# Attention issued two steps at a time: scores, value products and flips in pairs, gate products ahead

## The chip, the cores and the metric

The kernel runs on one core of one Trainium2 chip. The metric is the device time of one execution in microseconds. Five engines work side by side and meet at semaphores: TensorE (matrix products, PE in the profile, its weight loads PEld), VectorE (DVE), ScalarE (ACT), GpSimd (POOL) and SyncE (SP), whose queue issues most of the loads.

## The reference

Three parts, each fed by the one before:

```python
# attention: q, k, v of (2, 8, 576, 64)
scores = scale * np.matmul(q, k.transpose(0, 1, 3, 2))
mask_local = (rel >= 0) & (rel < 32)                              # heads 0 to 3
mask_strided = (rel >= 0) & (pos[None, :] % 32 == pos[:, None] % 32)   # heads 4 to 7
attn = exp(scores - max); attn = attn / (sum + 1e-09)
x = matmul(attn, v), as (1152, 512)

# mixture 1: 8 experts, one for each token (argmax of gate logits)
logits = x @ w_gate + modality_bias[modality_id]
out[mask] = gate_w[mask, None] * (relu(x[mask] @ w1[e]) @ w2[e])

# mixture 2: 4 experts, all of them for each token, weighted
out += p[:, e:e + 1] * (relu(x @ w1[e]) @ w2[e])
```

## The kernel before

Attention is cut into 22 steps, 11 for each of two batches. A step covers four heads. Steps 0 to 4 of a batch are the strided heads: 126 queries by 126 keys of seven residues (72 by 72 in the fifth). Steps 5 to 10 are the local heads: 96 queries by 128 keys. One step goes through the engines like this:

- TensorE, `score(i)`: a mask product (L1412) fills one of three banks (1, 2, 3 in turn), then the products of queries and keys (L1417, two passes for each of four heads) add to it. It waits until the exponentials of step i-3 are done.
- VectorE: the maximum of each row (L993) and its negation (L995).
- ScalarE: four exponentials with their sums (L675) into one of four buffers `prob`.
- VectorE, `invert(m)`: sum plus 1e-9 (L944), reciprocal (L947).
- GpSimd: probabilities times the reciprocal (L509).
- TensorE, `flip_prob(m)`: four transposes (L1430) into bank 4 (even steps) or 5 (odd steps). ScalarE copies even ones out (`keep_prob`, L664), VectorE odd ones (L956). Each flip waits for the copy of the flip two steps before.
- TensorE, `weigh(m)`: value products (L1456), 64 columns of weights for each head, so that two heads write the lower and the upper half of the partitions of bank 6 or 7. VectorE copies the result to `xT` (`keep_att`, L979 and L984).

In the loop before (L1460 to L1468) each turn i issues the scores of step i, the flip of step i-3 (`LAG_T`) and the value products of step i-5 (`LAG_V`). The same order is written out by hand for the other engines: VectorE (L987 to L1015) takes the maximum of step i, then inverts the sum of step i-1, copies a flip if it is an odd one, copies the attention of step i-5. ScalarE (L666 to L681) copies an even flip, then takes the exponentials of step i.

Into this loop the kernel weaves the start of mixture 1. Once the tokens of tile t (128 tokens) are complete, the gate products of the tile (`gate_logits`, L1377, eight columns) are issued ahead of the value products of the same step, and a flip of the tile to token rows (`flip_rows`, L1372) behind them; `FLIP_AT` gives the step: tiles 0 to 3 at m = 8, 9, 10, 12. After step 10 VectorE finds the experts of the first three tiles, and at step 11 TensorE counts ranks (L1381 to L1393) and VectorE chooses the expert that is worked on first (`choose_first`). SyncE then asks for its weights (L388, L394), which ScalarE cuts (L650) right behind its last exponentials, ahead of the copy of flip 20. GpSimd scatters the rows of the three tiles (L503) behind the scalings of steps 17, 18 and 19; when all three have landed, SyncE loads the first tile of tokens of that expert (L408), and TensorE flips it (`flip_x`, L1499).

The remaining flips, value products and gate products (tiles 4 and 5) are written out behind the loop (L1470 to L1487). Ahead of the loop TensorE runs `WARM` = 8 products of ones (L1359). After attention come mixture 1 (L1522, L1536) and mixture 2 (L1612, L1641), which the change doesn't touch.

Of the kernel before, what the change touches and what calls it, by code (L numbers as in the profile page):

```python
# [40 lines left out]
def moe_chain(nc, qT_in, kT_in, v_in, modality_id, w_gate, modality_bias, w1, w2, domain_probs, u1, u2, out):  # L41
# [41 lines left out]
        return P if is_local(n) else residues(n) * PER_RES  # L83

    STEPS = B * TILES
    WARM, FIRST_TILES = 8, 2
    FIRST_COLS = FIRST_TILES * P_RES
    assert FIRST_TILES < STRIDED
    LAG_T, LAG_V = 3, 5
    PB = 4  # L90
    SCORE_BANKS = (1, 2, 3)

    def steps_before(t):

        b, at = divmod(P * (t + 1) - 1, S)
        return b * TILES + STRIDED + at // LQ + 1
# [1 line left out]

    GROUPS = ((0, 3), (3, 6), (6, 9))
    LOOP_TILES = GROUPS[1][0] + 1  # L100
    FLIP_AT, step = {}, 2 * STRIDED - 3
    for t in range(LOOP_TILES):
        step = max(step + (2 if t == 3 else 1), steps_before(t) + 1)
        FLIP_AT[step] = t
    FOUND_AT = max(step for step, t in FLIP_AT.items() if t < GROUPS[0][1])
    CHOSEN_AT = FOUND_AT + 1
    SCATTER_FROM = CHOSEN_AT + LAG_V + 1
    assert GROUPS[2][1] == NT and LOOP_TILES + 2 == GROUPS[1][1] and SCATTER_FROM + GROUPS[0][1] < STEPS

    ROW_BANK = [0] * LOOP_TILES + [2] * 3 + [1, 2]  # L110
# [49 lines left out]
    with ctx:  # L160
# [482 lines left out]
        def _(act):  # L643
# [19 lines left out]
                src = bank[4][:].rearrange("p (h r) -> p h r", h=HALF_H)  # L663
                a.copy(probT[0:C, 0, :, 0:R], src[0:C, :, 0:R]).then_inc(prob_kept_a, 1)  # L664

            for i in range(STEPS):  # L666
                m = i - LAG_T
                if m >= 0 and m % 2 == 0:
                    keep_prob(m)
                R, C, s = rows(i % TILES), keys(i % TILES), i % PB  # L670
                act.wait_ge(max_known, i + 1)
                if i >= PB:
                    act.wait_ge(prob_flipped, i - PB + 1)
                for h in range(HALF_H):
                    last = a.activation(prob[0:R, s, h, 0:C], bank[SCORE_BANKS[i % 3]][0:R, P * h:P * h + C], ACT.Exp,  # L675
                                        bias=neg_max[0:R, s, h:h + 1], scale=SCALE,
                                        accum_out=row_sum[0:R, s, h:h + 1])
                last.then_inc(exped, 1)
                t = FLIP_AT.get(i - LAG_V, 1)
                if t % 2 == 0:  # L680
                    keep_rows(t)  # L681

# [166 lines left out]
        def _(dve):  # L849
# [108 lines left out]
            def keep_att(m):  # L958

                b, n = divmod(m, TILES)  # L960
                R = rows(n)
                dve.wait_ge(weighed, m + 1)
                if m in FLIP_AT:
                    t = FLIP_AT[m]
# [22 lines left out]
            for i in range(STEPS):  # L987
                if i == TILES + 2:
                    small_steps()
# [7 lines left out]
                if i >= 1:  # L997
                    invert(i - 1)
                m = i - LAG_T
                if m >= 0 and m % 2:  # L1000
                    keep_prob(m)
                m = i - LAG_V
                if m >= 0:
                    keep_att(m)
                if m == FOUND_AT:
                    dve.wait_ge(vstep, st.value)
                    find_experts(slice(*GROUPS[0]))
                if m == CHOSEN_AT:
                    choose_first()
                if m == CHOSEN_AT + 1:  # L1010
                    find_slots(slice(*GROUPS[0]))
                if m == CHOSEN_AT + 2:
                    place_first()
                if FLIP_AT.get(m, 0) % 2:
                    keep_rows(FLIP_AT[m])  # L1015

            keep_prob(STEPS - 3)
            keep_att(STEPS - 5)
            invert(STEPS - 1)
            keep_att(STEPS - 4)  # L1020
# [3 lines left out]
            find_experts(slice(*GROUPS[1]))  # L1024
            keep_prob(STEPS - 1)
            for m in range(STEPS - 3, STEPS):
                keep_att(m)


            def keep_xt(j):  # L1030
# [324 lines left out]
        def _(pe):  # L1355
# [78 lines left out]
            def weigh(m):  # L1434

                b, n = divmod(m, TILES)
                R, C = rows(n), keys(n)
                pe.wait_ge(prob_kept_v if m % 2 else prob_kept_a, m // 2 + 1)
                if n == 0 or n == STRIDED:
                    pe.wait_ge(v_read[b][is_local(n)], 16)  # L1440
                if m >= 2:
                    pe.wait_ge(att_kept, m - 1)
                if m in FLIP_AT:
                    pe.wait_ge(gate_in, 16)
                    gate_logits(FLIP_AT[m], bank[6 + m % 2][:, P * 2:P * 2 + E])
# [8 lines left out]
                for h in range(HALF_H):  # L1454
                    o = D * (h % 2)
                    last = t_.matmul(bank[6 + m % 2][o:o + D, P * (h // 2):P * (h // 2) + R],  # L1456
                                     v_rows[0:C, m, h, :], probT[0:C, m % 2, h, 0:R], start=True, stop=True)
                last.then_inc(weighed, 1)

            for i in range(STEPS):  # L1460
                score(i)
                if i >= LAG_T:
                    flip_prob(i - LAG_T)
                m = i - LAG_V
                if m >= 0:
                    weigh(m)
                if m in FLIP_AT:
                    flip_rows(FLIP_AT[m], bank[0])  # L1468

            flip_prob(STEPS - 3)  # L1470
            weigh(STEPS - 5)
# [3 lines left out]
            flip_rows(LOOP_TILES, bank[ROW_BANK[LOOP_TILES]])  # L1475
            flip_prob(STEPS - 2)
            weigh(STEPS - 4)
            pe.wait_ge(att_kept, steps_before(LOOP_TILES + 1))
            gate_logits(LOOP_TILES + 1, bank[3][:, E:2 * E]).then_inc(logit_done, 1)
            flip_prob(STEPS - 1)  # L1480
            weigh(STEPS - 3)
            flip_rows(LOOP_TILES + 1, bank[ROW_BANK[LOOP_TILES + 1]])
            weigh(STEPS - 2)
            t0, t1 = GROUPS[1]
            pe.wait_ge(onehot_ready, 2)
            rank_group(t0, t1, bank[3][:, 2 * E:(2 + t1 - t0) * E]).then_inc(rank_done, 1)
            weigh(STEPS - 1)  # L1487


            def rank_last():  # L1490
# [259 lines left out]
```

## Time and profile before

| | |
|---|---|
| median of 3 runs | 608.01 us (607.55 to 608.05) |
| profiled execution | 611.28 us, span of the core 609.5 us |
| TensorE busy | 600.8 us, 99% of the span |
| VectorE, ScalarE, GpSimd busy | 347.3, 219.0, 300.8 us |
| attention on TensorE | from 5.27 to about 62 us |

A row of the timeline gives start, duration, engine, line, operation, what it writes and reads, the count, and in brackets the idle time before it and what ended that. A row of the chain of work that ended last gives start, duration and what. A row of a stretch gives its bounds and length, then for each engine the busy time and the number of instructions, the granted clock of TensorE (1.00 is 2.4 GHz, 0.50 is 1.2 GHz), the busy share of the DMA engines and GB/s.

### The profile page before, as it was taken

What the parts mean: (1) busy time and instruction counts of PE and PEld (TensorE: products, weight loads), DVE (VectorE), ACT (ScalarE), POOL (GpSimd) and SP (SyncE); (2) the same over time, 40 slices, a digit from 0 to 9 for tenths busy, and PEclk for the clock granted to TensorE, in tenths of its full rate; (3) what the DMA queues carried; (4) which work ended last, traced back from release to release, by engine and by line L of the source; (5) the groups of instructions that cost most, each with busy time, mean ns of one, the idle gap of its engine ahead of it and who ended that gap; (6) DMA issues with size and microseconds to landing.
All of it is one profiled execution on the core that took longest, in us unless ns stands there. A gap on an engine that the chain in (4) does not pass through costs nothing.

```text
span 609.5 us, 10253 instructions
## 1 busy us (share of the span) xinstructions
PE 600.8 (99%) x3615; PEld 527.5 (87%) x3616; DVE 347.3 (57%) x714; ACT 219.0 (36%) x543; POOL 300.8 (49%) x286
## 2 busy tenths in 40 slices
PE   8999999999999999999999999999999999999996
PEld 6898878888878889989889899899899899899894
DVE  6888775248882123785454554554554554654553
ACT  7867532258973231223123123122132132131130
POOL 5537301541100009449996945846756747646005
PEclk9999799999999999999999999999999999999999
DMA  8817446629951002002222112112112011020004
GB/s 233 226 47 277 159 174 238 210 84 306 351 221 30 24 17 70 1 0 70 70 69 71 35 35 69 36 35 69 33 36 69 24 45 60 12 65 0 0 0 155
DMA packets 25116, 56.83 MB, mean 93 GB/s; under 512 B 6784, under 2 KB 7808, under 8 KB 25088
## 3 DMA queue, kind: packets, MB, share of 16 engines
q1 hardware_dynamic: 16656, 32.06, 15.9%
q0 software_dynamic: 6848, 21.52, 10.9%
q10 hardware_dynamic: 1584, 2.88, 1.6%
q8 instruction: 16, 0.26, 0.2%
q14 instruction: 12, 0.10, 0.1%
HBM read 49.10 MB, written 7.36 MB: 93 GB/s over the span
## 4 chain that ended last, share of the span: by engine, by line
PE 86%; DMA 3%; DVE 3%; POOL 3%; issue 2%; ACT 1%; DVEq 0%; SPq 0%; ACTq 0%; POOLq 0%
PE bank L1641 30%; PE bank L1612 30%; PE bank L1522 8%; PE bank L1536 8%; PE bank L1417 2%; DMA w_raw<-in_moe_w 2%; POOL out L637 1%; PE bank L1456 1%; PE bank L1377 1%; PE bank L1511 1%; PE bank L1430 1%; PE bank L1372 1%; DVE w_lo L937 1%; PE bank L1499 1%; PE bank L1412 1%
## 5 line engine op out<-in xcount | busy, mean ns | idle before, releaser
L1277 DVE SCALAR_TENSOR_TENSOR acc<-bank,meta_s,acc 128x512 f32<-128x512 f32 x135 | 100.8, 748 | 62.2 <-PE bank L1641 62.1
L1641 PE MATMUL bank<-u_hi,h_hi 128*128 128x512 f32 x288 | 112.3, 390 | 0.0
L1641 PE MATMUL bank<-u_lo,h_hi 128*128 128x512 f32 x288 | 112.1, 389 | 0.0
L1641 PE MATMUL bank<-u_hi,h_lo 128*128 128x512 f32 x288 | 112.0, 389 | 0.0
L1324 DVE SCALAR_TENSOR_TENSOR h_lo<-bank,h_hi 128x288 fp32r<-128x288 f32 x112 | 50.9, 455 | 44.7 <-ACT h_hi L825 22.9
L1612 PE MATMUL bank<-x2T_hi,u_hi 128*128 128x288 f32 x232 | 68.4, 295 | 0.0
L1612 PE MATMUL bank<-x2T_lo,u_hi 128*128 128x288 f32 x232 | 68.4, 295 | 0.0
L1612 PE MATMUL bank<-x2T_hi,u_lo 128*128 128x288 f32 x232 | 68.3, 295 | 0.0
L813 ACT COPY part_p<-bank 128x288 f32<-128x288 f32 x28 | 11.2, 400 | 157.9 <-PE bank L1612 157.9
L1612 PE MATMUL bank<-t_hi,u_hi 128*128 128x288 f32 x224 | 66.2, 295 | 0.0
L1612 PE MATMUL bank<-t_lo,u_hi 128*128 128x288 f32 x224 | 66.0, 295 | 0.0
L1612 PE MATMUL bank<-t_hi,u_lo 128*128 128x288 f32 x224 | 65.9, 294 | 0.0
L1641 PEld LDWEIGHTS bank<-u_hi,h_lo 128*128 128x128 f32 x288 | 54.1, 188 | 11.4
L1641 PEld LDWEIGHTS bank<-u_hi,h_hi 128*128 128x128 f32 x288 | 54.1, 188 | 10.1
L1641 PEld LDWEIGHTS bank<-u_lo,h_hi 128*128 128x128 f32 x288 | 54.1, 188 | 10.0
L584 POOL TENSOR_TENSOR u_lo<-u_raw,u_hi 128x1792 fp32r<-128x1792 f32 (+1 forms) x16 | 61.6, 3852 | 1.3
L574 POOL TENSOR_TENSOR u_raw<-u_raw 128x256 f32<-128x256 f32 x14 | 10.3, 735 | 87.7 <-PE bank L1612 71.0
L554 POOL DMA_INDIRECT meta_by_rank<-meta,pos x9 | 11.5, 1273 | 84.2 <-ACT y_tile L710 61.9
L582 POOL CAST u_hi<-u_raw 128x1792 fp32r<-128x1792 f32 (+1 forms) x16 | 25.6, 1601 | 41.3 <-PE bank L1612 38.2
L1612 PEld LDWEIGHTS bank<-x2T_hi,u_hi 128*128 128x128 f32 x232 | 43.5, 188 | 0.7 <-issue 0.2
L1612 PEld LDWEIGHTS bank<-x2T_lo,u_hi 128*128 128x128 f32 x232 | 43.5, 188 | 0.6
L1612 PEld LDWEIGHTS bank<-x2T_hi,u_lo 128*128 128x128 f32 x232 | 43.5, 188 | 0.0
(237 smaller groups left out, 1234.0 us busy)
## 6 DMA issues: line engine op xcount, KB each, us to landing
w_raw<-in_moe_w SPq DMA_DIRECT2D x20, 1024.0 KB, 8.5
u_raw<-in_moe_w POOLq DMA_DIRECT2D x16, 512.0 KB, 3.8
u_raw<-in_moe_w POOLq DMA_DIRECT2D x16, 256.0 KB, 3.2
u_raw<-in_moe_w POOLq DMA_DIRECT2D x32, 128.0 KB, 2.9
x_tile<-x_by_expert ACTq DMA_DIRECT2D x11, 256.0 KB
x_by_expert<-zero_row SPq DMA_DIRECT2D x10, 256.0 KB, 2.7
qT<-in_qT SPq DMA_DIRECT2D x3, 576.0 KB, 6.3
kT<-in_kT SPq DMA_DIRECT2D x6, 288.0 KB, 7.3
```

The source lines that it names most:

```text
L554: pool.indirect_dma_start(out=ms, out_offset=bass.IndirectOffsetOnAxis(ap=pos[:, t:t + 1], axis=0), in_=meta[:, t, :], in_offset=None).the ...
L574: g.tensor_tensor(u1_raw[:, S1], u1_raw[:, A21], u1_raw[:, A22], ALU.add).then_inc(u_summed, 1)
L582: g.tensor_copy(u1_hi[n % 2][:, need], u1_raw[:, need]).then_inc(u1_hi_cut, 1)
L584: g.tensor_tensor(u1_lo[n % 2][:, need], u1_raw[:, need], u1_hi[n % 2][:, need].bitcast(FP32), ALU.subtract)\
L813: a.copy(part[s][k][:], bank[s][:, 0:SUB]).then_inc(part_kept[s], 1)
L1277: w.scalar_tensor_tensor(out=acc[:, t, :], in0=bank[Z_BANK[i]][:], scalar=meta_s[:, t, bass.ds(e + 1, 1)], in1=acc[:, t, :], op0=ALU.mult, ...
L1324: w.scalar_tensor_tensor(out=h_lo[:, i, cols_of(s, k)], in0=bank[at][:, 0:SUB], scalar=0.0, in1=h_hi[:, i, cols_of(s, k)].bitcast(FP32), o ...
L1417: last = t_.matmul(bank_s[0:R, h, 0:C], qT[:, b, c, q0:q0 + R], kT[:, b, h % 2, c, k0:k0 + C], start=False, stop=True, skip_group_check=True)
L1522: last = t_.matmul(bank[half][:], lhs[:, c, :], rhs[:, c, HALF * half:HALF * (half + 1)], start=c == 0 and lhs is xt_hi and rhs is w1_hi, ...
L1536: last = t_.matmul(bank[5][:], lhs[:, f, :], rhs[:, f, :], start=f == 0 and rhs is w2_hi and lhs is ht_hi, stop=f == FCH - 1 and lhs is ht_lo)
L1612: last = t_.matmul(bank[at][:, 0:SUB], lhs_part[page][:, lhs, c, :], rhs[:, c, :], start=start and c == 0 and i == 0, stop=c == KC - 1 and ...
L1641: last = t_.matmul(bank[Z_BANK[i]][:], lhs[:, c, ts], rhs[page][:, c, :], start=c == 0 and k == 0, stop=c == 1 and k == 2)
```

## The change

Everything in the attention loop goes by two steps. TensorE issues the scores of steps i and i+1, then the gate products of steps m and m+1 (m = i-4), then the value products of both, then the flip of a tile to rows if one is due, then the flips of steps i-2 and i-1. `LAG_T` becomes 2, `LAG_V` 4. In the turn with m = 0 the two flips stand between the scores of steps 4 and 5. VectorE takes the maxima of steps i and i+1 first, then copies and inverts; ScalarE takes the exponentials of both, then copies an even flip. Gate products have steps of their own (`GATE_AT`: tiles 0 to 3 at 8, 9, 10, 12), flips to rows others (`ROWS_AT`: 8, 10, 12, 14). The ranks of the first group move from step 11 to step 12, the scatters stay behind the scalings of steps 17 to 19. `WARM` becomes 10.

```diff
-    WARM, FIRST_TILES = 8, 2
+    WARM, FIRST_TILES = 10, 2
-    LAG_T, LAG_V = 3, 5
+    LAG_T, LAG_V = 2, 4
...
+    CHOSEN_AT = FOUND_AT - FOUND_AT % 2 + 2
...
 (ScalarE)
+            for i in range(0, STEPS, 2):
+                exponential(i)
+                exponential(i + 1)
+                if i >= LAG_T:
+                    keep_prob(i - LAG_T)
+                t = ROWS_AT.get(i - LAG_V, 1)
                 if t % 2 == 0:
                     keep_rows(t)
...
 (VectorE)
+            for i in range(0, STEPS, 2):
+                find_max(i)
+                find_max(i + 1)
                 m = i - LAG_V
+                if m == min(GATE_AT) - min(GATE_AT) % 2:
+                    small_steps()
                 if m >= 0:
                     keep_att(m)
+                if m == CHOSEN_AT:
+                    choose_first()
+                invert(i)
+                if m >= 0:
+                    keep_att(m + 1)
+                if i >= LAG_T:
+                    keep_prob(i - LAG_T + 1)
+                invert(i + 1)
+                if m == FOUND_AT - FOUND_AT % 2:
                     dve.wait_ge(vstep, st.value)
                     find_experts(slice(*GROUPS[0]))
                 if m == CHOSEN_AT:
                     find_slots(slice(*GROUPS[0]))
                     place_first()
...
 (TensorE)
+            for i in range(0, STEPS, 2):
+                m = i - LAG_V
                 score(i)
+                if m == 0:
                     flip_prob(i - LAG_T)
+                    flip_prob(i - LAG_T + 1)
+                score(i + 1)
                 if m >= 0:
+                    if m >= 2:
+                        pe.wait_ge(att_kept, m)
+                    gates(m)
+                    gates(m + 1)
                     weigh(m)
+                    weigh(m + 1)
+                if m in ROWS_AT:
+                    flip_rows(ROWS_AT[m], bank[0])
+                if i >= LAG_T and m != 0:
+                    flip_prob(i - LAG_T)
+                    flip_prob(i - LAG_T + 1)
+
             pe.wait_ge(exped, STEPS - 1)
             pe.wait_ge(att_kept, steps_before(LOOP_TILES))
             gate_logits(LOOP_TILES, bank[3][:, 0:E])
             pe.wait_ge(att_kept, steps_before(LOOP_TILES + 1))
             gate_logits(LOOP_TILES + 1, bank[3][:, E:2 * E]).then_inc(logit_done, 1)
+            flip_prob(STEPS - 2)
+            flip_rows(LOOP_TILES, bank[ROW_BANK[LOOP_TILES]])
+            weigh(STEPS - 4)
+            weigh(STEPS - 3)
             flip_prob(STEPS - 1)
             flip_rows(LOOP_TILES + 1, bank[ROW_BANK[LOOP_TILES + 1]])
             weigh(STEPS - 2)
+            weigh(STEPS - 1)
```

## Rows read from the trace of the kernel before

**Rows 1.** Busy time by stretch, behind attention.
```profile
100.00:150.00 50.00, 50.00 (x250) 40.95 (x249) 24.38 (x28) 27.13 (x41) 18.63 (x18) 1.00 0.67 225
```

**Rows 2.** Chain of work that ended last, one local step.
```profile
26.46 0.48 PE bank L1456 x8
26.94 0.36 PE bank L1412
27.30 0.88 PE bank L1417 x8
28.18 0.33 PE bank L1430 x4
```

**Rows 3.** The same chain, other widths, gate products and a flip of rows.
```profile
22.37 0.58 PE bank L1456 x8
...
24.50 0.40 PE bank L1456 x8
...
32.60 0.82 PE bank L1377 x8
...
33.91 0.59 PE bank L1372 x4
34.49 0.21 PE bank L1412
```

**Rows 4.** The same chain at the start of attention.
```profile
9.78 0.69 DVE row_max L993
...
10.70 1.51 ACT prob L675 x8
...
12.69 1.04 POOL prob L509
...
18.76 0.35 PE bank L1412
```

**Rows 5.** Timeline at the start, ScalarE and VectorE.
```profile
8.57 0.37 ACT L675 ACTIVATE prob<-bank,neg_max 126x126 f32<-126x126 f32 x1 [2.47 <-DVE neg_max L995]
...
12.12 0.37 ACT L675 ACTIVATE prob<-bank,neg_max 126x126 f32<-126x126 f32 x1
...
12.53 0.65 DVE L993 TENSOR_REDUCE row_max<-bank 126x4 f32<-126x504 f32 x1
...
13.50 0.59 ACT L664 COPY probT<-bank 126x504 f32<-126x504 f32 x1
```

**Rows 6.** Timeline of TensorE at the start.
```profile
1.03 3.59 PE L1359 MATMUL bank<-ones 128*128 128x512 bf16 x8 [1.03 <-POOL ones L449]
5.27 0.65 PE L1412 MATMUL bank<-mask_res,ident_b 126*126 126x504 bf16 x1 [0.64 <-DMA kT<-in_kT]
5.71 1.91 PE L1417 MATMUL bank<-kT,qT 128*126 128x126 f32 x8
...
9.95 1.08 PE L1417 MATMUL bank<-kT,qT 128*126 128x126 f32 x8
```

**Rows 7.** Granted clock by stretch, last but two columns, end of attention.
```profile
64.00:65.00 1.00, 1.00 (x8) 0.97 (x8) 1.00 (x2) 0.34 (x1) 0.84 (x1) 0.82 1.02 389
...
71.00:72.00 1.00, 1.00 (x11) 0.63 (x11) 0.00 (x0) 1.00 (x2) 0.00 (x0) 0.77 0.00 0
```

**Rows 8.** Timeline at the end of attention, all engines.
```profile
55.21 0.55 PE L1430 MATMUL bank<-ident,prob 96*128 96x96 f32 x4 [0.46 <-POOL prob L509]
...
55.32 1.01 POOL L503 DMA_INDIRECT x_by_expert<-xtok,slot  x1 [0.17 <-issue]
...
61.12 0.36 SPq L408 DMA_DIRECT2D x_tile<-x_by_expert  x1
...
63.55 0.96 PE L1377 MATMUL bank<-gate,xT 128*128 128x8 f32 x8
...
64.16 1.09 POOL L503 DMA_INDIRECT x_by_expert<-xtok,slot  x1 [2.94 <-DMA x_tile<-x_by_expert]
...
65.23 1.06 PE L1499 MATMUL bank<-ident,x_tile 128*128 128x128 f32 x4
```

More of the change, by code:

```diff
@@ L100, in moe_chain @@
     LOOP_TILES = GROUPS[1][0] + 1
-    FLIP_AT, step = {}, 2 * STRIDED - 3
+    GATE_AT, ROWS_AT, step = {}, {}, STRIDED
     for t in range(LOOP_TILES):
[L103 to L106, printed above, removed]
+        step = step + 1
+        while step - step % 2 < steps_before(t):
+            step = step + 1
+        GATE_AT[step] = t
+    for t in range(LOOP_TILES):
+        first = min(step for step, u in GATE_AT.items() if u == t)
+        ROWS_AT[max(first - first % 2, max(ROWS_AT, default=0) + 2)] = t
+    FOUND_AT = max(step for step, t in GATE_AT.items() if t < GROUPS[0][1])
+    CHOSEN_AT = FOUND_AT - FOUND_AT % 2 + 2
     SCATTER_FROM = CHOSEN_AT + LAG_V + 1
+    assert STEPS % 2 == 0 and STRIDED == LAG_V + 1
     assert GROUPS[2][1] == NT and LOOP_TILES + 2 == GROUPS[1][1] and SCATTER_FROM + GROUPS[0][1] < STEPS
@@ L664, in keep_prob, with exponential @@
                 a.copy(probT[0:C, 0, :, 0:R], src[0:C, :, 0:R]).then_inc(prob_kept_a, 1)
[L666 to L669, printed above, removed]
+            def exponential(i):
                 R, C, s = rows(i % TILES), keys(i % TILES), i % PB
@@ L678, in _ @@
                 last.then_inc(exped, 1)
-                t = FLIP_AT.get(i - LAG_V, 1)
+            for i in range(0, STEPS, 2):
[4 more added lines that the diff above has]
+                t = ROWS_AT.get(i - LAG_V, 1)
                 if t % 2 == 0:
@@ L962, in keep_att @@
                 dve.wait_ge(weighed, m + 1)
-                if m in FLIP_AT:
-                    t = FLIP_AT[m]
+                if m in GATE_AT:
+                    t = GATE_AT[m]
                     w.tensor_tensor(logits[:, t, :], bank[6 + m % 2][:, P * 2:P * 2 + E], bias_tok[:, 0, t, :],
@@ L985, in keep_att, with find_max @@
                     last.then_inc(att_kept, 1)
-            for i in range(STEPS):
-                if i == TILES + 2:
-                    small_steps()
+            def find_max(i):
                 R, C, s = rows(i % TILES), keys(i % TILES), i % PB
@@ L996, in _ @@
                  .then_inc(max_known, 1)
[L997 to L1001, printed above, removed]
+            for i in range(0, STEPS, 2):
+                find_max(i)
+                find_max(i + 1)
                 m = i - LAG_V
+                if m == min(GATE_AT) - min(GATE_AT) % 2:
+                    small_steps()
                 if m >= 0:
                     keep_att(m)
-                if m == FOUND_AT:
+                if m == CHOSEN_AT:
[7 more added lines that the diff above has]
+                if m == FOUND_AT - FOUND_AT % 2:
                     dve.wait_ge(vstep, st.value)
@@ L1008, in _ @@
                 if m == CHOSEN_AT:
-                    choose_first()
-                if m == CHOSEN_AT + 1:
                     find_slots(slice(*GROUPS[0]))
-                if m == CHOSEN_AT + 2:
                     place_first()
[L1014 to L1020, printed above, removed]
+                if ROWS_AT.get(m, 0) % 2:
+                    keep_rows(ROWS_AT[m])
             dve.wait_ge(logit_done, 1)
@@ L1024, in _ @@
             find_experts(slice(*GROUPS[1]))
+            keep_att(STEPS - 4)
+            keep_att(STEPS - 3)
             keep_prob(STEPS - 1)
-            for m in range(STEPS - 3, STEPS):
-                keep_att(m)
+            keep_att(STEPS - 2)
+            keep_att(STEPS - 1)
             def keep_xt(j):
@@ L1442, in weigh, with gates @@
                     pe.wait_ge(att_kept, m - 1)
-                if m in FLIP_AT:
+                for h in range(HALF_H):
+                    o = D * (h % 2)
+                    last = t_.matmul(bank[6 + m % 2][o:o + D, P * (h // 2):P * (h // 2) + R],
+                                     v_rows[0:C, m, h, :], probT[0:C, m % 2, h, 0:R], start=True, stop=True)
+                last.then_inc(weighed, 1)
+            def gates(m):
+                if m in GATE_AT:
                     pe.wait_ge(gate_in, 16)
-                    gate_logits(FLIP_AT[m], bank[6 + m % 2][:, P * 2:P * 2 + E])
+                    gate_logits(GATE_AT[m], bank[6 + m % 2][:, P * 2:P * 2 + E])
                 if m == CHOSEN_AT:
@@ L1453, in weigh @@
                     count_group(t1, bank[6 + m % 2][:, at:at + E])
[L1454 to L1460, printed above, removed]
+            for i in range(0, STEPS, 2):
+                m = i - LAG_V
                 score(i)
-                if i >= LAG_T:
+                if m == 0:
                     flip_prob(i - LAG_T)
-                m = i - LAG_V
+                    flip_prob(i - LAG_T + 1)
+                score(i + 1)
                 if m >= 0:
+                    if m >= 2:
+                        pe.wait_ge(att_kept, m)
+                    gates(m)
+                    gates(m + 1)
                     weigh(m)
[L1467 to L1471, printed above, removed]
+                    weigh(m + 1)
[4 more added lines that the diff above has]
+                    flip_prob(i - LAG_T + 1)
             pe.wait_ge(exped, STEPS - 1)
@@ L1474, in _ @@
             gate_logits(LOOP_TILES, bank[3][:, 0:E])
-            flip_rows(LOOP_TILES, bank[ROW_BANK[LOOP_TILES]])
-            flip_prob(STEPS - 2)
-            weigh(STEPS - 4)
             pe.wait_ge(att_kept, steps_before(LOOP_TILES + 1))
             gate_logits(LOOP_TILES + 1, bank[3][:, E:2 * E]).then_inc(logit_done, 1)
+            flip_prob(STEPS - 2)
+            flip_rows(LOOP_TILES, bank[ROW_BANK[LOOP_TILES]])
+            weigh(STEPS - 4)
+            weigh(STEPS - 3)
             flip_prob(STEPS - 1)
-            weigh(STEPS - 3)
             flip_rows(LOOP_TILES + 1, bank[ROW_BANK[LOOP_TILES + 1]])
             weigh(STEPS - 2)
+            weigh(STEPS - 1)
             t0, t1 = GROUPS[1]
@@ L1486, in _ @@
             rank_group(t0, t1, bank[3][:, 2 * E:(2 + t1 - t0) * E]).then_inc(rank_done, 1)
-            weigh(STEPS - 1)
             def rank_last():
```

## The prediction

> **What bounds the kernel now.** I read the busy time by stretch first, then the chain of work that ended last, then the timelines of the stretches that the change touches, then the granted clock. In the stretch from 100 to 150 us TensorE is busy for all of it [rows 1], the first of ten such stretches up to 600 us, which read alike, so a microsecond won before is won at the end. Attention covers 5.3 to some 62 us. There TensorE is busy without a break from 14 to 54 us. It waits at the start, where the first softmax has to run through VectorE, ScalarE and GpSimd, and once at 55.2 us, for 0.46 us, for GpSimd [rows 8]. So two things decide: what TensorE needs for a pair of steps, and whether the other engines keep up with the new order.
>
> **What a step costs.** In the chain a step without gate work is mask product, score products, flip, value products: 0.36 + 0.88 + 0.33 + 0.48 = 2.05 us [rows 2]. Value products take 0.40 us for 72 columns, 0.48 for 96 and 0.58 for 126 [rows 2, 3]. That is a line of 3.3 ns a column with 0.16 us left at zero columns: a fixed cost on entering them. The mask product takes 0.36 us behind value products [rows 2] but 0.21 behind a flip of rows (the row at 34.49, [rows 3]): 0.14 to 0.15 for leaving them. Value products write halves of the partitions (64 columns of weights each), all else uses the full width. By the Trainium skill, page "TensorEngine Tiling (Array Packing)", section "Tiling Modes", a change of tiling mode drains the engine. The trace agrees as far as it goes: 0.16 us in and 0.14 out. If that rule alone were at work, two value products of one mode in a row would share one drain.
>
> **The change part by part.**
> 1. Pairs of value products. Before, 22 steps each enter and leave: 22 x 0.30. After, 11 pairs do: 11 x 0.30 = **3.3 us saved** on TensorE. No row shows two value products of different steps in a row, so the bounds are 0 (the cost is one of a step, not of a mode) and 3.3. I take 3.3, since eight products of one step with alternating halves show no such cost among themselves.
> 2. Start, at the clock of before. VectorE now takes the maxima of two steps and then inverts two sums. The second inversion waits for the exponentials of step 1, and the maximum of step 2 is queued behind it. Exponentials of step 1 start at 10.70 and are done at 12.21; the inversion ends at about 12.53, which is when the maximum of step 3 started before [rows 4, 5]. So now the maximum of step 2 starts at 12.53. With 0.69 + 0.18 + gaps, exponentials of step 2 start at 13.45 (before 12.12), those of step 3 1.42 later at 14.87 (the spacing 10.70 to 12.12), and are done at 16.4. Only then does ScalarE copy the first flip out (0.59, [rows 5]), which flip 2 needs: flip 2 runs 16.9 to 17.35. GpSimd scales step 3 from 16.75 to 17.8 (1.04, [rows 4]), flip 3 (0.43) ends at 18.3, scores of step 5 at 19.35, value products 0 and 1 (0.16 + 0.42 + 0.42) at 20.35. Before, the value products of step 1 ended at 18.76 with the scores of step 6 (0.35 + 0.88) done too, thus 17.53 for the same work [rows 4]. Start costs 2.8, and one saved mode change is in it: **3.1 us of waits added**. Bounds 2.3 to 3.6, by whether the copy of the first flip really ends the wait.
> 3. Middle. VectorE and ScalarE form a loop now: maximum and negation 0.88, exponentials of two steps 1.42 + 1.51, inversion 0.3, and only then the next maximum: 4.1 us a pair. TensorE needs 2 x (0.21 + 0.88 + 0.32 + 0.33) + 0.30 = 3.8 for a pair without gate work. So the pairs gain less than they seem to, as long as they run on the slack between score and flip; pairs with gate products and flips of rows (0.82 + 0.59 more, [rows 3]) refill it. No wait taken here.
> 4. End. In the iteration of step 16 VectorE does ranks, slots and places of the first group, and the maximum of step 18 is queued behind. Count from the end of scores 17, as estimates from the durations above: value products 12 end at 1.7, VectorE has copied and chosen by 3.3, inverted 16 and 17 and copied by 4.9, and is free at 6.1. Exponentials 18 run 7.0 to 8.4, 19 to 9.9; TensorE has ended scores 21 at 9.8 and wants flip 19 at about 11.7, when the scaling of 19 is held by that of 18 and a scatter (1.0 + 1.2 on GpSimd) until 12.1. So 0.4 of waiting; then 0.3 for exponentials 20 before the gate product that uses the scores' bank, and 0.2 for a copied row tile: 0.9, against the 0.46 of before [rows 8], which goes. **0.45 added**, bounds -0.5 to 1.2.
> 5. The first token tile. Its load is issued at 61.12, after the third scatter (issued 55.32) has landed, GpSimd sees it at 64.16, and TensorE reaches its flip at 65.23 [rows 8]: 1.1 us of slack. The scatters keep their place behind the scaling of steps 17 to 19. These come some 1.0 to 1.5 us later by parts 2 and 4, so the tile becomes the last to arrive: **0.3 added**, bounds 0 to 1. The expert's weights are asked for later as well, by the same delay. On ScalarE the first cut of them stands ahead of the copy of flip 20, so a late weight would hold value products 20. The trace of before shows ScalarE never waiting there, so I put it at nothing; it is in the upper bound.
> 6. Gate products ahead of the value products, flips behind: the same instructions in another place, inside the count of part 1; the mode changes are the same. Zero.
> 7. Ten products of ones. Eight run from 1.03 for 3.59 us at 0.43 us each, half clock, and TensorE then sits for 0.64 us until keys arrive at 5.27 [rows 6]. Two more fill just that hole and end at 5.3 to 5.5: nothing is delayed by more than 0.2. The level granted here is read from the durations: products of step 0 take 1.91 us for eight, those of step 2 only 1.08 from 9.95 on [rows 6]. So the engine went from 1.2 to 2.4 GHz near 9.9, after work without a break from 5.27. Without the hole it works without a break from 1.03, and the rise may come sooner: at best before the first score (5.3), at worst at 9.9 as now. I take 6.5, in the scores of step 0. They end 0.64 sooner, exponentials of step 0 start at 7.93 instead of 8.57 [rows 5], those of step 1 1.42 later, at 9.35 instead of 10.70: **1.3 saved**, bounds 0 and 1.9 (all scores at 2.4 GHz).
> 8. The clock in the new lull. By part 2 TensorE has, between the scores of step 4 and flip 3, some 3 us with one flip of 0.43 in it. In the trace the clock falls to 0.50 in the stretch 64 to 65 and is back in 71 to 72: some 6.8 us at 1.2 GHz, worth 3.4 [rows 7]. What TensorE did before that fall shows as busy, but the most of it is gate products with eight columns each, 0.96 us for a tile [rows 8]. The lull is thinner than that. Its price lies between 0 (no fall, or a slow stretch that ends with the lull) and 3.4 (one like that at the end, all under dense work). I take a fall that costs about half of it, since a part lies in the waits: **1.6 added**.
>
> Sum: -3.3 + 3.1 + 0.45 + 0.3 - 1.3 + 1.6 = **+0.85 us**. The profiled execution took 611.28 us with a span of 609.5, the median of the runs is 608.01. The profiled one should go to about 612.1, the median to **608.85**.
>
> **The rivals.**
> A. The clock rises early and stays: the same sum without part 8, 608.85 - 1.6 = 607.25. For it: there are some short flips in the lull. Against: the lull holds fewer columns than the stretch before 64.7.
> B. Slower: no early rise (eight products of ones, 3.59 us without a break, didn't bring it, and two more may not, [rows 6]) and a fall in the lull: 608.85 + 1.3 = 610.15. It decides as soon as products of step 1 still take 1.7 us and those of step 5 twice 0.88. Without rise and without fall it is 608.55.
> C. The fall at the end goes. The slow stretch at the end costs 3.4 [rows 7]. With attention packed more closely around 61 to 64 us it may be kept: 605.45. Against: products for the gate of tiles 6 and 7 stand where they stood, and in the new tail two more stand side by side.
> D. The change doesn't do what it says: entering and leaving cost something per step, and half of the 3.3 stays: 608.85 + 1.65 = 610.5.
>
> **How the numbers follow.** Forecast 0.33, A 0.26, B with fall 0.12, neither rise nor fall 0.08, C 0.14, D 0.07. Stalls of parts 2, 4 and 5 are known to about 0.8 us around each. 0.2% is 1.2 us, about what a measurement of this kernel can tell from no change. Slower than 609.2: a third of the forecast, B, D and a little of the others, 0.33. Faster than 606.8: C and a third of A, 0.24. The rest, 0.43, within. The range goes from 606.2 (A with its spread) to 610.6 (B and D), which leaves out C and little else.
>
> **What would show it.** Mode changes: the mask product of odd steps at 0.21 and one entry cost for each pair. Start: TensorE waits between the scores of step 4 and flip 3, over 2 us in all, released by ScalarE's copy and by GpSimd, and VectorE's maximum of step 2 starts behind the inversion of step 1. Clock: products of step 1 near 0.9 us for eight (early rise), scores of steps 5 to 7 near twice their time (fall). End: the flip of the first token tile released by its load. If the waits at the start come to less than 1.5 us, or the clock is high from 6.5 to 64 us, I am wrong on the slow side.

## The result and the profile after

The changed kernel takes **615.57 us** in the median of four executions (614.62 to 616.23), the kernel before 607.78 beside it: a ratio of 1.0123, 95% interval 1.0103 to 1.0143. It is slower by 7.8 us, where 608.85 and a range up to 610.6 were forecast. The profiled execution took 614.62 us with a span of 612.9. TensorE is busy for 597.9 us, 98% of the span, against 600.8 and 99% of a shorter one; VectorE, ScalarE and GpSimd are busy for about as long as before (350.6, 217.8, 301.6 us).

TensorE's waits up to 75 us, of the kernel after. The columns are the engine, what it wrote, the line, what ended the wait, then the sum in us, how often, and the longest; `issue` means that the profile shows nothing that the engine waited for.

```profile
PE bank L1443 <- ACT probT L670: 2.2, 1, 2.2
PE bank L1443 <- POOL prob L515: 1.8, 4, 0.7
PE bank L1425 <- ACT prob L679: 1.3, 1, 1.3
PE bank L1458 <- issue: 1.1, 3, 0.5
...
PE bank L1390 <- ACT prob L679: 1.0, 1, 1.0
PE bank L1425 <- DMA kT<-in_kT: 0.4, 1, 0.4
```

These six come to 7.8 us. The same view of the kernel before has only two, beside the 1.0 us for the ones that both kernels have:

```profile
PE bank L1430 <- POOL prob L509: 0.8, 2, 0.5
PE bank L1412 <- DMA kT<-in_kT: 0.6, 1, 0.6
```

So 6.4 us of waits came in, and the saving in mode changes (3.3) pays half of them. The start, on TensorE's timeline after (it answers to [rows 6]):

```profile
1.03 4.45 PE L1372 MATMUL bank<-ones 128*128 128x512 bf16 x10 [1.03 <-POOL ones L455]
...
5.70 1.18 PE L1430 MATMUL bank<-kT,qT 128*126 128x126 f32 x8
...
12.29 0.65 PE L1443 MATMUL bank<-ident,prob 126*126 126x126 f32 x4 [0.67 <-POOL prob L515]
...
15.80 0.69 PE L1443 MATMUL bank<-ident,prob 126*126 126x126 f32 x4 [2.21 <-ACT probT L670]
16.76 1.10 PE L1443 MATMUL bank<-ident,prob 126*126 126x126 f32 x4 [0.27 <-POOL prob L515]
...
18.08 1.80 PE L1430 MATMUL bank<-kT,qT 128*96 128x128 f32 x8
```

The products of the first score take 1.18 us where they took 1.91: the clock rose early. Flip 2 waits 2.21 us for ScalarE's copy, as forecast. The products of 18.08 take 1.80, twice the 0.88 of [rows 2]: the clock has fallen. The end, on the same timeline (it answers to [rows 8]):

```profile
56.77 0.42 PE L1425 MATMUL bank<-mask_local,ident_b 96*96 96x512 bf16 x1 [1.27 <-ACT prob L679]
...
58.57 0.88 PE L1458 MATMUL bank<-probT,v_rows 128*64 128x96 f32 x16 [0.51 <-issue]
...
60.55 0.55 PE L1443 MATMUL bank<-ident,prob 96*128 96x96 f32 x4 [0.62 <-POOL prob L515]
62.11 1.95 PE L1390 MATMUL bank<-gate,xT 128*128 128x8 f32 x16 [1.01 <-ACT prob L679]
...
72.01 0.60 PE L1523 MATMUL bank<-ident,x_tile 128*128 128x128 f32 x4
```

Four waits of 3.41 us stand where there was one of 0.46, and the flip of the first token tile starts at 72.01 instead of 65.23. Granted clock by stretch, after (columns as in [rows 7]):

```profile
17.00:18.00 1.00, 1.00 (x5) 0.93 (x5) 0.00 (x0) 1.00 (x8) 0.00 (x0) 0.50 1.19 226
...
64.00:65.00 1.00, 1.00 (x7) 1.00 (x7) 0.83 (x3) 0.75 (x1) 1.00 (x2) 0.50 0.92 369
65.00:66.00 1.00, 1.00 (x10) 0.67 (x10) 0.58 (x4) 0.00 (x0) 0.91 (x4) 0.50 0.11 41
```

There are two slow stretches, from about 16.2 to 19.6 us and from 64.0 to 67.4. Besides, every profile of this study, before and after, is at 0.50 in the last 1 to 4 us of its span.

**A quantity for what follows.** How long the clock stays low differs between executions of one kernel, so I set two numbers beside each time: the granted clock, averaged over the span, and the span times that clock. The product takes out what the low clock adds and leaves work and waits. It is a rough tool: the clock is given to three digits, which is 0.3 us either way; where TensorE waits at the low clock it takes out too much; and the slow products of ones at the start are still in it, since the clock reads 1.00 there. Medians:

| kernel | executions | time, us | clock | span x clock, us |
|---|---|---|---|---|
| before (beside the first experiments) | 31 | 608.65 | 0.997 | 605.2 |
| after | 4 | 615.57 | 0.992 | 608.9 |

The kernel after wasn't repeated; the four executions of before beside it had a median of 607.78. Of the 7 us or so between the two rows, 3.7 are work and waits (6.4 of waits less 3.3 of mode changes is 3.1), and the rest, some 3.2, is the lower clock: 613.8 x 0.008 = 4.9 us against 606.9 x 0.003 = 1.8.

### The profile page after: what moved, and what is told of

Its sections match the earlier page's. It is cut to its first block, busy times and chain, and to the rows that moved or that the text cites. A ratio compares the mean times of both kernels' runs of the same rounds, so it can differ in the third digit from the quotient of the medians.

```text
span 612.9 us, 10261 instructions
## 1 busy us (share of the span) xinstructions
PE 597.9 (98%) x3617; PEld 525.7 (86%) x3618; DVE 350.6 (57%) x714; ACT 217.8 (36%) x543; POOL 301.6 (49%) x286
## 4 chain that ended last, share of the span: by engine, by line
PE 88%; DVE 4%; ACT 2%; POOL 2%; issue 1%; DMA 1%; SPq 0%; POOLq 0%
PE bank L1665 30%; PE bank L1636 29%; PE bank L1560 10%; PE bank L1546 10%; ACT prob L679 2%; PE bank L1535 2%; POOL out L643 1%; PE bank L1430 1%; PE bank L1458 1%; PE bank L1523 1%; DVE row_max L1002 1%; PE bank L1529 1%; PE bank L1443 1%; PE bank L1372 1%; PE bank L1390 1%
```

## The experiments

**The kernel before, once more.** Unchanged.

> The kernel before once more, unchanged, for a second profile and the span and clock of several executions. The median of the runs of before is 3.3 us under its profiled execution (608.0 against 611.3). Theory 'slow tail': the profiled one had a stretch at 1.2 GHz behind attention (64 to 72 us, worth 3.4 us) that most executions don't have; then this profile, or most of its runs, shows a span near 606 and a clock above 0.995. Rival 'profiling costs it': the span is 609.5 again with the same slow stretch.

Measured: 608.88 us, ratio 1.0005 (0.998 to 1.003), and a profile with a span of 606.1 us, 3.4 less than the profiled execution that the prediction was worked from. The two stretches of [rows 7] and the flip of the token tile read:

```profile
64.00:65.00 1.00, 1.00 (x10) 0.97 (x10) 1.00 (x2) 0.31 (x1) 0.73 (x1) 1.00 0.97 365
71.00:72.00 1.00, 1.00 (x6) 0.81 (x5) 0.99 (x2) 0.86 (x2) 0.73 (x1) 1.00 0.00 0
...
64.92 0.60 PE L1499 MATMUL bank<-ident,x_tile 128*128 128x128 f32 x4
```

The slow tail that I took for a fixed cost of the kernel (3.4 us, part 8 and rival C) is absent here. Two thirds of the executions of before have a clock of 0.996 or more. So the 3.3 us between the profiled 611.28 and the median 608.01 were mostly this stretch.

**Ten products of ones alone** (kernel before with `WARM = 10`).

```
-    WARM, FIRST_TILES = 8, 2
+    WARM, FIRST_TILES = 10, 2
```

> The kernel before with ten products of ones instead of eight, nothing else. Theory of the forecast: the clock rises in the scores of step 0, the first exponentials start 0.7 to 1.3 us sooner, and the whole kernel gains 1.3: ratio 0.998. Rival: the loads of queries and keys hold the third score, and the start is given back: ratio 1.000.

Measured: 607.55 us, ratio 0.9974 (0.9952 to 0.9996); span x clock 604.2. A gain of 1.0 us by span x clock and 1.6 by the ratio, against 1.3 forecast: part 7 is right as far as this can tell, the interval being 0.2 to 2.9 us. In the profiled execution the products of each of the first four scores take 1.04 us, and the third waits 0.95 us for its keys (the first 0.66: the hole of part 7 isn't filled, as the ten products of ones take only 4.07 us there), so only part of the early rise comes through. It is the fastest kernel of the study, by little more than can be told.

**The second inversion behind the next pair's first maximum** (kernel after).

```
                 find_max(i)
+                if i >= 2:
+                    invert(i - 1)
                 find_max(i + 1)
...
-                invert(i + 1)
...
+            invert(STEPS - 1)
```

> The changed kernel; VectorE takes the second inversion of a pair behind the first maximum of the next pair, so the maximum no longer waits for the exponentials. Theory 'loop' (VectorE and ScalarE go round in 4.1 to 4.5 us a pair): the waits in the middle and half of those at the start and the end go, 3 to 4 us of 7.8; about 612. Rival 'clock' (the loss is slow stretches): 615.5, with the same slow stretches in the profile.

Measured: 609.83 us, ratio 1.0021 (0.9999 to 1.0044); span x clock 605.1, clock 0.9955. This one move takes 5.7 us off the median (6.2 by the ratios), where 3 to 4 and a time of 612 were expected. Of them 3.8 are work and waits, as expected for the loop; the other 2 are clock (0.9955 against 0.992). VectorE in the middle of attention, after:

```profile
22.74 0.66 DVE L1002 TENSOR_REDUCE row_max<-bank 96x4 f32<-96x512 f32 x1
23.43 0.53 DVE L1004 TENSOR_SCALAR neg_max<-row_max 96x4 f32<-96x4 f32 x1
...
26.91 0.17 DVE L954 TENSOR_SCALAR row_sum<-row_sum 96x4 f32<-96x4 f32 x1
27.20 0.65 DVE L1002 TENSOR_REDUCE row_max<-bank 96x4 f32<-96x512 f32 x1
```

The maximum of 27.20 starts 4.46 us after that of 22.74, right behind the second inversion (from 26.91), which waits for exponentials that wait for the maximum before: a closed loop, which I had put at 4.1. ScalarE is idle in it 1.2 to 1.3 us a pair. The missing 0.36 is one small operation, at 23.43, that takes 0.53 instead of 0.17. It ends at 23.96, and GpSimd's scaling that was under way ends at 22.90 + 1.04 = 23.94: it didn't run slowly but was held until the scaling was done. GpSimd's scalings show this and the period, first after and then with the deferred inversion:

```profile
22.90 1.04 POOL L515 TENSOR_TENSOR prob<-prob,row_inv 96x512 f32<-96x512 f32 x1 [0.61 <-DVE row_inv L957]
...
25.98 1.04 POOL L515 TENSOR_TENSOR prob<-prob,row_inv 96x512 f32<-96x512 f32 x1 [2.04 <-DVE row_inv L957]
...
30.44 1.04 POOL L515 TENSOR_TENSOR prob<-prob,row_inv 96x512 f32<-96x512 f32 x1 [2.04 <-DVE row_inv L957]
```

```profile
25.85 1.04 POOL L515 TENSOR_TENSOR prob<-prob,row_inv 96x512 f32<-96x512 f32 x1 [1.10 <-DVE row_inv L957]
...
29.87 1.04 POOL L515 TENSOR_TENSOR prob<-prob,row_inv 96x512 f32<-96x512 f32 x1 [1.28 <-DVE row_inv L957]
```

The period of 4.46 became 4.02, and the wait of 2.21 at the start became 0.83.

**Ten more products of ones in the lull** (kernel after; ahead of flip 2).

```
                 if m == 0:
+                    for _ in range(10):
+                        t_.matmul(bank[7][:].rearrange("p (h c) -> p h c", h=HALF_H), ones[:],
+                                  ones[:].unsqueeze(1).to_broadcast([P, HALF_H, P]), start=True, stop=True)
                     flip_prob(i - LAG_T)
```

> The changed kernel with ten more products of ones (0.21 us each) between the scores of step 4 and the flip of step 2, where TensorE waits 2.2 us. Theory 'clock falls in the lull': the level stays at 1.00 from 16 to 20 us and 1.6 us come back, about 614. Rival: the clock falls whatever the lull holds, or another fall takes its place: 615.5.

Measured: 614.94 us, ratio 1.0084 (1.0049 to 1.012); span x clock 608.7 as without them, clock 0.9935 against 0.992. In the profile the granted clock is 1.00 in every stretch from 14 to 22 us, so the fall in the lull is gone. The second slow stretch stays. The times tell its price badly: 0.6 us by the medians, 0.9 by the clock (613.8 x 0.0015), 2.4 by the ratios (1.0084 against 1.0123), with six executions that spread over 2.9 us. The two profiles tell more. GpSimd's scalings of steps 3 and 4, after and then with the filled lull:

```profile
15.68 1.03 POOL L515 TENSOR_TENSOR prob<-prob,row_inv 126x504 f32<-126x504 f32 x1 [0.36 <-DVE row_inv L957]
21.62 0.67 POOL L515 TENSOR_TENSOR prob<-prob,row_inv 72x288 f32<-72x288 f32 x1 [4.92 <-DVE row_inv L957]
```

```profile
16.11 1.03 POOL L515 TENSOR_TENSOR prob<-prob,row_inv 126x504 f32<-126x504 f32 x1 [0.36 <-DVE row_inv L957]
20.65 0.67 POOL L515 TENSOR_TENSOR prob<-prob,row_inv 72x288 f32<-72x288 f32 x1 [3.52 <-DVE row_inv L957]
```

Step 3 is 0.43 us later with the filled lull (keys came later), step 4 is 0.97 earlier: the fall costs 1.4 us here, and 0.95 of the lead is still there at the last scaling (62.98 against 63.93). This execution then loses 1.0 us to loads of weights in mixture 1, which stand on its chain of work at 153 and 166 us and not on that of the kernel after. Part 8 was right that the lull brings a fall, and its price of 1.6 fits the profiles; the medians can't settle it.

**Slots and places behind the next pair's maxima** (kernel after).

```
                 find_max(i + 1)
                 m = i - LAG_V
+                if m == CHOSEN_AT + 2:
+                    find_slots(slice(*GROUPS[0]))
+                    place_first()
...
-                if m == CHOSEN_AT:
-                    find_slots(slice(*GROUPS[0]))
-                    place_first()
```

> The changed kernel with slots and places of the first group taken one iteration later on VectorE, behind the maxima of steps 18 and 19. Theory 'queue': in the changed kernel these stand 2.3 us ahead of the maximum of step 18, and the waits of TensorE before scores 21 (1.27) and value products 16 (0.51) come from them; they go, 1.2 to 1.8 us, span times clock 607.3 instead of 608.9. Rival 'loop only' (VectorE and ScalarE set the pace anyway): under 0.5 us.

Measured: 616.63 us, ratio 1.011 (1.0045 to 1.0176); span x clock 607.55, 1.35 below after and near the expected 607.3, but clock 0.9875. In the profile the wait of 1.27 is gone and a flip waits 1.20 instead of 0.62, so the waits at the end sum to 2.72 instead of 3.41; the wait of 0.51, which was expected to go, stays. Where the rest of the 1.35 comes from isn't shown. A longer slow stretch (61 to 71 us) took more than that back. By the time alone one would have called the move useless.

**Both deferrals**, twice, on two occasions.

> Both edits on VectorE: second inversion behind the next maximum, and slots and places one iteration later. If the two causes add, span times clock is 1 us under that of the deferred inversion alone (605.1): 604.1, and the ratio to before about 0.999. Rival: with the loop gone the slots hide already, no difference to the deferred inversion alone.

Measured: 610.42 us, ratio 1.0018 (0.9984 to 1.0051), span x clock 604.9. Second occasion:

> The changed kernel with both deferrals, once more, on the chip of the two kernels with the extra products of ones: 610.4 as before, granted clock 0.994 in the median. If the clock of its executions is 0.997 or more here, the fall depends on the chip and the hour and the two kernels beside it say nothing on its cause.

Measured: 611.12 us, 1.0039 (1.002 to 1.0058), 605.1. Beside the deferred inversion alone (605.1) the slots give nothing, as the rival had it. Work and waits are back at those of before (604.4 to 605.2), and what is left of 2.5 to 3 us is the clock, 0.993 to 0.994 against 0.997. But back at before isn't below it: the 3.3 us saved on mode changes and the 1.0 of the early rise are still eaten by waits. In the first profile TensorE waits for other engines or keys for 4.5 us up to 75 us (0.70, 0.82, 0.69 and 1.06 at flips among them), against 1.4 before. So even with both deferrals the change gains nothing.

**A tiny full-width product between two value products** (both deferrals, nine pairs).

```
                     weigh(m)
+                    t_.matmul(bank[6 + (m + 1) % 2][:, 480:488], ones[:], ones[:, 0:8], start=True, stop=True)
                     weigh(m + 1)
```

> The kernel with both VectorE edits, and in each of the nine pairs of value products inside the loop one product of ones with 8 columns at full width between the two steps. Theory 'mode': each breaks a pair and brings back 0.30 us plus 0.03 for itself, 9 x 0.33 = 3.0 us where TensorE has no wait to hide it, 2 us or more in all. Rival 'cost per step': the two value products paid their 0.16 separately already, and only some 0.3 us are added in all.

Measured: 610.89 us, ratio 1.0046 (1.0019 to 1.0073); span x clock 605.6, so 0.7 above the same kernel without it, where 2 or more were expected. The chain of work shows the price itself, first without and then with the product, both at 96 columns:

```profile
29.71 0.81 PE bank L1460 x16
```

```profile
29.47 0.48 PE bank L1460 x8
29.95 0.11 PE bank L1491
30.07 0.48 PE bank L1460 x8
```

Sixteen value products take 0.81, or 0.48 + 0.11 + 0.48 = 1.07 with a product of eight columns between: some 0.27 more a pair with the small product's own time in it, 2.4 for nine, and 0.48 is what a step cost before [rows 2]. Only 0.7 of that reaches the end. The rest went into waits for GpSimd, as far as the profiles show: TensorE's weight loads wait 4.8 us for scalings up to 57 us in both profiles without the products and 2.9 with them, and the two flips behind the pair shown take 0.81 us with and 1.02 without.

**The second tile's gate products behind two value products** (both deferrals).

```
             gate_logits(LOOP_TILES, bank[3][:, 0:E])
-            pe.wait_ge(att_kept, steps_before(LOOP_TILES + 1))
-            gate_logits(LOOP_TILES + 1, bank[3][:, E:2 * E]).then_inc(logit_done, 1)
...
             weigh(STEPS - 3)
+            pe.wait_ge(att_kept, steps_before(LOOP_TILES + 1))
+            gate_logits(LOOP_TILES + 1, bank[3][:, E:2 * E]).then_inc(logit_done, 1)
```

On VectorE the copies of value products 18 and 19 go ahead of the logits to fit.

> Both VectorE edits, and in the written-out end the gate products of tile 5 stand behind value products 18 and 19 instead of right behind those of tile 4, with the two copies ahead of the logits on VectorE. Theory 'thin stretch': the clock falls at 60 us because two gate products stand side by side with waits around them; spread out it falls less often, more of the runs have a clock of 0.996 or more than with both edits alone, median 1 us lower. Rival: the falls come from the flips of rows and gate products of tiles 6 to 8, where nothing is changed: same share of low clocks.

Measured: 617.33 us, ratio 1.0107 (1.0064 to 1.015), and a span x clock of 604.8, the same as without the move. The clock is 0.982. Its profile is at half clock from about 57.6 to 78 us, of which this is one stretch:

```profile
70.00:71.00 1.00, 1.00 (x6) 1.00 (x7) 0.00 (x0) 0.33 (x1) 0.93 (x1) 0.50 0.67 258
```

The time is some 7 us longer with span x clock unchanged: the clock alone moves this kernel as far as the whole change did. That the clock falls less when these thin products are spread out is refuted for this order.

**Products of ones in the waits at the end** (both deferrals, on the second occasion). Four of 512 columns between flips 18 and 19; the second kernel has six more of 384 columns between the gate products of the two tiles.

```
                     flip_prob(i - LAG_T)
+                    if i == STEPS - 2:
+                        for _ in range(4):
+                            t_.matmul(bank[5][:].rearrange("p (h c) -> p h c", h=HALF_H), ones[:],
+                                      ones[:].unsqueeze(1).to_broadcast([P, HALF_H, P]), start=True, stop=True)
                     flip_prob(i - LAG_T + 1)
...
             gate_logits(LOOP_TILES, bank[3][:, 0:E])
+            for _ in range(6):
+                t_.matmul(bank[3][:, P:].rearrange("p (h c) -> p h c", h=3), ones[:],
+                          ones[:].unsqueeze(1).to_broadcast([P, 3, P]), start=True, stop=True)
```

> The changed kernel with both deferrals (inverses and slots behind the next pair's first maximum), and four extra products of ones of 512 columns (0.22 us each, 0.88 in all) in the wait of 1.06 us that TensorE has between the flips of steps 18 and 19. Question: is the slow stretch from about 58.5 to 62 us brought on by TensorE's waits just ahead of it? If the waits bring it on: the granted clock stays at 1.00 from 57 to 63 us, the median of the granted clock rises from 0.994 to 0.998, and the time falls by 1.5 to 2 us against the same kernel without them, to some 608.5. If the gate products with eight columns bring it on, and not the waits: same clock, time the same or up to 0.3 later.

Measured: 609.75 us, 1.0028 (1.001 to 1.0046), clock 0.996 in the median against 0.993 without. Against the kernel without the products the clock rose by 0.003 and the time fell by 1.4 us, where 0.004 and 1.5 to 2 were expected if the waits bring the fall on, and nothing if they don't.

> As the one with four products, and six more products of ones of 384 columns (0.16 us each, about 1.0 us) between the gate products of the first and of the second tile behind attention. If waits or thin gate products bring the clock down, it stays at 1.00 from 57 to 66 us; the six products stand on the path, so the time is 608.5 + 1.0 = 609.5 where the four alone suffice, and still some 609.5 (against 610.4 without either) where only both together keep the clock. If the fall has nothing to do with what TensorE does there: the slow stretch is as long as before, and the time is 610.4 + 1.0 = 611.4.

Measured: 609.92 us (609.18 to 610.4), 1.0008 (0.9983 to 1.0033), clock 0.997. All ten executions are at 0.996 or more; of the same kernel without the products, on the same chip, not one of ten is. Span x clock rose from 605.1 to 606.4, the 1.0 us of the six products, and still the median fell from 611.12 to 609.92. The two sets of clocks don't overlap (0.997 to 0.999 against 0.992 to 0.995); the times do (609.18 to 610.4 against 609.33 to 612.08). TensorE by stretch, in the kernel with neither, with four, with ten; the columns are the bounds, length, busy time and count of TensorE, granted clock, DMA share, GB/s:

```profile
55.00:57.00 2.00, 0.93 (x13) 1.00 0.98 323
57.00:59.00 2.00, 2.00 (x18) 0.80 1.01 365
59.00:61.00 2.00, 2.00 (x12) 0.50 1.01 386
...
63.00:65.00 2.00, 2.00 (x16) 0.50 0.16 24
```

```profile
55.00:57.00 2.00, 1.80 (x17) 1.00 0.95 322
57.00:59.00 2.00, 2.00 (x21) 1.00 1.00 356
...
67.00:69.00 2.00, 2.00 (x13) 0.81 1.05 408
69.00:71.00 2.00, 2.00 (x8) 0.50 0.60 233
```

```profile
57.00:59.00 2.00, 2.00 (x18) 1.00 1.03 360
...
69.00:71.00 2.00, 2.00 (x28) 1.00 0.56 210
```

Without them TensorE waits half of the two microseconds from 55 to 57 and the clock falls at once behind. With the wait filled it doesn't fall there. With four alone it falls later, near 68; with ten not at all in this execution.

## Why the prediction was wrong

The forecast was +0.85 us and the time moved by some 7. Three steps failed. Part 3 took no wait for the loop of VectorE and ScalarE. Part 4, which should have inherited the loop's lag, put 0.45 us where the waits at the end grew by 2.95. And part 8 with the sum carried the slow stretch at the end as something that doesn't change, though the median of before hasn't got it and the kernel after has.

**Part 1, mode changes: right.** The value products of two steps of 126 columns enter once (1.01 = 0.16 + 0.84), and the mask product of an odd step takes 0.22 instead of 0.36. From the chain of work after:

```profile
20.89 0.35 PE bank L1425
21.24 0.87 PE bank L1430 x8
22.11 0.22 PE bank L1425
22.33 0.87 PE bank L1430 x8
23.20 1.01 PE bank L1458 x16
```

The tiny product shows that a pair saves its price only while nothing of full width stands inside, so rival D falls; the price by it is up to 0.27 a pair, where 0.30 was taken. The Trainium skill, page "TensorEngine Tiling (Array Packing)", section "Tiling Modes", has the rule of a drain at a change of mode; the trace agrees: 0.27 us more a pair once a product of another width stands between.

**Part 2, start: right.** The flips wait 0.26 + 0.67 + 2.21 + 0.27 = 3.41 us; the flip of step 1 waited 0.30 before (0.8 for the flips in the waits of before, less the 0.46 of [rows 8]). That is 3.1 more, as forecast, and the longest is the one for the copy of the first flip.

**Part 3, middle: wrong, and the step that matters most.** The loop of VectorE and ScalarE was seen, and its 4.1 us a pair set beside TensorE's 3.8, with the words "No wait taken here". It takes 4.46. In the middle itself that costs only 0.15 + 0.43 us of waits, but each pair uses up slack between score and flip, so VectorE comes late to the end. From 44.4 us to 56.7, where its queue is full of work on experts and slots, it shows no wait and yet takes the maximum of step 18 3.2 us after that score is done (at 51.05); with the inversion deferred it takes it 1.0 us after (48.86). After, then deferred:

```profile
54.21 0.68 DVE L1002 TENSOR_REDUCE row_max<-bank 96x4 f32<-96x512 f32 x1
```

```profile
49.90 0.68 DVE L1002 TENSOR_REDUCE row_max<-bank 96x4 f32<-96x512 f32 x1
```

The failure was to price a closed loop as slack and not to carry its lag (0.66 us a pair: 4.46 less TensorE's 3.8) into part 4, and to sum the loop from durations of undisturbed operations, though the trace of before has slow ones too (0.53 us for the negation at 13.21). The Trainium skill, page "Trainium Architecture — The Big Picture", section "What this means for kernel authors", says that VectorE and GpSimd share a port under an exclusive lock. The trace agrees: 0.17 us alone, 0.53 when started inside a scaling, and ended with it.

**Part 4, end: places right, size wrong.** Of the three waits named, that for scaling 19 takes 0.62 (0.4 forecast), that for exponentials 20 takes 1.01 (0.3), and the copied row tile isn't waited for (0.2). Not foreseen were 1.27 of the scores of step 21 for exponentials 18, and 0.51 ahead of value products 16. Together 3.41 against 0.9. With the inversion deferred, what remains is one wait of about 0.4 and one of 0.67, so most of 3.41 was the lag of part 3. The queue of slots, which part 4 did name, is behind 0.7 of it in the profile with the slots moved.

**Part 5, token tile: no.** Its first flip doesn't wait for the load after the change. TensorE itself came 6.8 us later.

**Part 6:** nothing seen against it. **Part 7: right**, 1.0 to 1.6 us, with the reservation above.

**Part 8, clock: half right.** The fall in the lull came, at 16.2, and costs about what was forecast (1.4 us in the profiles, 0.6 to 2.4 by the times, 1.6 forecast). The fall at the end was treated as one that stays the same (worth 3.4, and it might go, rival C). It isn't in the median of before (clock 0.997; the profile without the fall has 0.998), and the four executions after the change all have the clock of the profiled one, 0.992, which has two falls. So the sum, made against the profiled 611.28 and then shifted to the median, carried the tail as a constant when it was what changed.

**The miss in sum.** 615.57 is 6.7 above the forecast, 0.6 of which is that before itself had 608.65 in the longer series instead of 608.01. The forecast had +0.85 = -0.75 of work and waits (part 7 with them) + 1.6 of clock; measured are 3.7 and 3.2. So some 4.4 us of the miss are work and waits and 1.6 clock, each to about half a microsecond. The waits that the view lists explain 2.6 of the 4.4 (6.4 came in, and parts 2, 4 and 5 had 3.85). The other 1.8 aren't assigned to a part; short waits between the products of two flips, which the view doesn't list, are in it.

**Open.** With the waits near 55 to 60 us filled the clock stayed up in all ten executions, so what TensorE does there has a part in the fall. That doesn't tell how much of the waits and of the thin products is needed. The kernel before, whose wait there is 0.46 us, falls in some executions too (with ten products of ones ahead, at 59.4 and 66.0 us in the profile), and why the same instructions keep the clock in one execution and lose it in the next isn't known.

## What to carry to other kernels

When an edit lets one engine do work for two steps before it turns to the next pair, write the cycle of waits out as a loop, and count every operation on it at the duration that it has beside its neighbours; a loop slower than the engine that bounds the kernel uses up the slack pair by pair, and the wait comes where the pipeline drains. Before a sum is made against a profiled execution, compare it with the median of the runs, and where they differ, ask which stretch of low clock is in the one and not in the other. When work and waits (span x clock) and the time disagree, look at the clock first, and try a few products of ones in TensorE's waits.

## What the runs showed of the hardware

- The kernel before took between 606.2 and 613.4 us in 31 executions with span x clock within 602.6 to 606.5: about half of the range of 7.2 us, and most of the usual spread, is TensorE's clock (standard deviation 1.8 us of the span, 0.9 of the product).
- A wait of 1.06 to 1.07 us ahead of eight-column gate products was followed by 3.4 us at 1.2 GHz in one profile and 6.8 in another; four products of ones in that wait, 0.88 us of work, removed it there. The Trainium skill, page "TensorE: Matmul & The Clock Gate", section "HAM oscillation — how this bites in real kernels", tells of falls behind long waits for DMA; here the waits are short and for other engines.
- Small operations of VectorE (96x4, 126x4, 128x3) that start inside a scaling of GpSimd are held until it ends. They take 0.17 us alone and up to 0.81 beside one; one on slots takes 1.04 where it starts 0.01 us into a scaling, and 0.52 in the kernel before, where it starts 0.54 us into one. Up to 66 us of the kernel after, 14 such operations take over 0.25 us, and all 14 end within 0.04 us of the GpSimd operation that they started in. Not everything is held: four operations on 128x1 at 49.84 to 50.15 us of the kernel before take 0.14 to 0.20 inside a scaling of 49.19 to 50.23. Maxima, which read the scores' bank, keep their 0.65 to 0.69.
